# A gated scan, an up-projection by seven products and a down-projection: four kinds of GpSimd instruction at other places in its queue

## The reference, cut to what matters

```python
# x, f_logit: (2, 6080, 256)   lower_bound: (256,)   w_in: (256, 2048)   w_out: (2048, 256)
f = lower_bound + (1 - lower_bound) * sigmoid(f_logit)
h = f[:, t] * h + (1 - f[:, t]) * x[:, t]      # for t in range(6080); y[:, t] = h
u = y.reshape(12160, 256) @ w_in
g = where(u > 0, u, exp(min(u, 0)) - 1)        # ELU
out = g @ w_out                                # (12160, 256), float32
```

## Time and profile before

| | |
|---|---|
| median of 3 runs | 1010.96 us (1010.54 to 1011.62) |
| the profiled execution | 1011.16 us |
| its span in the profile | 1009.3 us |
| TensorE busy | 1003.2 us, 99% |
| ScalarE busy | 794.6 us, 79% |
| VectorE busy | 728.9 us, 72% |
| GpSimd busy | 632.9 us, 63% |
| TensorE's granted clock | full in all 40 slices |
| TensorE's share of the chain that ended last | 97% |
| GpSimd's low part of an operand made from `x` (L334), 33 of them | 1.16 / 1.30 / 1.76 us (least, median, most) |
| VectorE's `open_gate` (L584), longest | 1.56 us |
| GpSimd's idle time in block 0, ahead of ELU 30's low part | 5.60 us |
| distance of the same matmul in two blocks that follow each other | 83.34 us |

### The profile page before, as it was taken

One profiled execution on the slowest core, in us unless ns is written; L12 is line 12 of the kernel. 1 busy time (PEld: TensorE's weight loads), 2 busy tenths in 40 slices (PEclk: granted clock), 3 DMA queues, 4 the chain that ended last, 5 costly groups with the idle time before them and its releaser, 6 DMA issues.

```text
span 1009.3 us, 15356 instructions
## 1 busy us (share of the span) xinstructions
PE 1003.2 (99%) x4362; PEld 816.4 (81%) x4362; DVE 728.9 (72%) x913; ACT 794.6 (79%) x1427; POOL 632.9 (63%) x474
## 2 busy tenths in 40 slices
PE   8999999999999999999999999999999999999998
PEld 5788778888888888888888888888888888888997
DVE  6785886785787687688669669758867966875544
ACT  7997778877877777877787787787788778778775
POOL 2584897567557557656655755756675575566454
PEclk9999999999999999999999999999999999999999
DMA  7211102101201110210120120021021011000101
GB/s 271 63 32 43 54 1 74 53 1 52 73 0 32 41 51 0 73 52 0 55 70 0 42 60 24 6 66 52 0 62 62 0 42 60 12 0 5 40 1 37
DMA packets 23211, 41.88 MB, mean 41 GB/s; under 512 B 2704, under 2 KB 4240, under 8 KB 23184
## 3 DMA queue, kind: packets, MB, share of 16 engines
q1 hardware_dynamic: 22752, 41.04, 12.7%
q10 hardware_dynamic: 432, 0.53, 0.2%
HBM read 29.10 MB, written 12.45 MB: 41 GB/s over the span
## 4 chain that ended last, share of the span: by engine, by line
PE 97%; DVE 1%; issue 1%; DMA 1%; ACT 0%; ACTq 0%; DVEq 0%
PE acc L858 17%; PE acc L856 17%; PE acc L857 17%; PE h L828 14%; PE h L830 14%; PE h L832 13%; PE h L951 1%; PE h L952 1%; PE h L953 1%; DMA x<-value 1%; DVE x L599 0%; DVE x L591 0%; PE acc L952 0%; PE acc L953 0%; PE acc L951 0%
## 5 line engine op out<-in xcount | busy, mean ns | idle before, releaser
L314 POOL TENSOR_TENSOR g_lo<-e,g_hi 128x512 fp32r<-128x512 f32 (+1 forms) x384 | 517.3, 1356 | 370.7 <-ACT g_hi L452 370.4
L438 ACT ACTIVATE e<-h 128x512 f32<-128x512 f32 (+1 forms) x380 | 226.4, 596 | 163.6 <-PE h L832 128.3
L690 DVE SCALAR_TENSOR_TENSOR e<-e,h 128x512 f32<-128x512 f32 (+1 forms) x380 | 257.3, 677 | 80.0 <-ACT e L444 79.8
L858 PE MATMUL acc<-g_hi,w_out_lo 128*128 128x512 f32 (+1 forms) x768 | 301.9, 393 | 0.0
L856 PE MATMUL acc<-g_hi,w_out_hi 128*128 128x512 f32 (+1 forms) x768 | 301.0, 392 | 0.0
L857 PE MATMUL acc<-g_lo,w_out_hi 128*128 128x512 f32 (+1 forms) x768 | 299.7, 390 | 0.0
L452 ACT CAST g_hi<-e 128x512 fp32r<-128x512 f32 (+1 forms) x384 | 233.1, 607 | 22.3 <-DVE e L690 22.3
L444 ACT ACTIVATE e<-e 128x512 f32<-128x512 f32 (+1 forms) x384 | 242.1, 630 | 8.4
L828 PE MATMUL h<-a_hi,w_in_hi 128*128 128x512 f32 (+1 forms) x616 | 241.2, 392 | 0.3 <-DVE h L676 0.3
L830 PE MATMUL h<-a_lo,w_in_hi 128*128 128x512 f32 (+1 forms) x616 | 240.6, 391 | 0.0
L832 PE MATMUL h<-a_hi,w_in_lo 128*128 128x512 f32 (+1 forms) x616 | 238.8, 388 | 0.0
(11 more groups left out here) (64 smaller groups left out, 571.4 us busy)
## 6 DMA issues: line engine op xcount, KB each, us to landing
out<-out_sb SPq DMA_DIRECT2D x44, 256.0 KB, 2.1
gate<-forget_logit SPq DMA_DIRECT2D x43, 256.0 KB, 2.7
x<-value SPq DMA_DIRECT2D x43, 256.0 KB, 2.8
w_in_raw<-w_in SPq DMA_DIRECT2D x8, 256.0 KB, 6.4
w_out_raw<-w_out SPq DMA_DIRECT2D x8, 256.0 KB, 7.7
x<-value SPq DMA_DIRECT2D x4, 224.0 KB, 2.6
gate<-forget_logit SPq DMA_DIRECT2D x4, 224.0 KB, 2.5
out<-out_sb SPq DMA_DIRECT2D x4, 224.0 KB, 2.0
```

The lines of the kernel that those rows point to most:

```text
L314: nc.gpsimd.tensor_tensor(g_lo[:, t % RING, 0:w], e[:, t % TILES, 0:w], g_hi[:, t % RING, 0:w].bitcast(F32), ALU.subtract).then_inc(g_lo_r ...
L438: nc.scalar.activation(e[:, i, 0:w], bank_of(j, t)[:, 0:w], ACT.Relu, scale=-1.0).then_inc(r_ready, 1)
L690: nc.vector.scalar_tensor_tensor(e[:, t % TILES, 0:w], e[:, t % TILES, 0:w], -1.0, bank_of(j, t)[:, 0:w], ALU.add, ALU.max).then_inc(g_rea ...
L858: done = nc.tensor.matmul(bank, lo, g_hi[:, t % RING, 0:w], start=False, stop=closes)
```

## The change

Low part of the fourth operand: in every block from 1 on, GpSimd made it after the ELU low part of (q, i) = (0, C11) of the same block. Now it makes it after that of (7, C22) of the block before (t = 30), ahead of that of (7, C21).

Low parts of w_in for groups 2 to 7: the P1 to P3 pieces of groups 2 and 3 move from block 1 to block 0 (after t = 25 and 27), and the others take other places in block 1.

```diff
             def spare(j, par, q, i, last):
 
-                if (q, i) == (0, C11):
-                    rest(j, par, P4)
                 if last:
                     return
...
                     rest(j + 1, 1 - par, P6)
+                if (q, i) == (7, C22):
+                    rest(j + 1, 1 - par, P4)
 
             def second_spare(q, i):
 
                 at = (q, i)
-                if at in ((0, C12), (1, C11), (1, C22), (2, C12), (3, C12), (4, C12)):
-                    w_in_rest({(0, C12): 2, (1, C11): 3, (1, C22): 4, (2, C12): 5, (3, C12): 6, (4, C12): 7}[at],
-                              P1, P5)
-                if at in ((0, C22), (1, C12), (2, C11), (2, C22), (3, C22), (5, C12)):
-                    w_in_rest({(0, C22): 2, (1, C12): 3, (2, C11): 4, (2, C22): 5, (3, C22): 6, (5, C12): 7}[at],
+                if at in ((0, C22), (1, C12), (3, C22), (4, C21)):
+                    w_in_rest({(0, C22): 4, (1, C12): 5, (3, C22): 6, (4, C21): 7}[at], P1, P5)
+                if at in ((0, C11), (0, C12), (1, C11), (1, C22), (4, C12), (5, C12)):
+                    w_in_rest({(0, C11): 2, (0, C12): 3, (1, C11): 4, (1, C22): 5, (4, C12): 6, (5, C12): 7}[at],
                               P5, PRODUCTS)
...
                 rest_g(0, t)
                 if t in (18, 21):
                     rest(1, 1, {18: P1, 21: P2}[t])
+                if t in (25, 27):
+                    w_in_rest({25: 2, 27: 3}[t], P1, P5)
+                if t == 30:
+                    rest(1, 1, P4)
```

## The result

The changed kernel took 1009.52 us (median of 22 runs) where the kernel before took 1011.40 us beside it; the ratio is 0.9982, 95% interval 0.9975 to 0.9988. A second set of 11 runs gave 0.9983 (0.9974 to 0.9992). So the change wins 1.8 us of 1011, under 0.2%. Forecast were 1009.3 us and a gain of 1.64; "VectorE wins the race in group 2", the first rival, gave 1.91 and 1009.05. Both start from 1010.96 us, the median of three runs; the 22 runs beside the changed kernel have 1011.40. So the gains are to be compared and not the times. The interval, 1.2 to 2.5 us, holds 1.64 and 1.91 both: which of the two it was, only the trace tells.

What follows compares the result with a forecast made beforehand. TensorE, busy 99% of the span, bounds the kernel; only its waits can be won. 1.05 (fourth operand) + 0.59 (group 3 of block 1) = 1.64 us less, 1009.3 us against 1010.96; range 1008.5 to 1010.3.

Steps and rivals of the forecast that it cites:

- VectorE wins the race in group 2: Rival, block 1: VectorE's `weigh` begins ahead of GpSimd's ELU 7, so all 1.91 us go; 1009.05 us, chance 0.30.
- The ten waits are GpSimd's low part of the fourth operand: Ahead of P4 in group 0, blocks 1 to 10: TensorE's unnamed waits are for this GpSimd subtraction; moving it gives -1.05 us.
- It fits the idle time of 1.60 us and moves nothing: Steady blocks: the moved subtraction takes 1.30, at most 1.48, inside GpSimd's idle time before ELU 31; nothing behind it moves.
- Two pieces into block 0 cost nothing: Block 0: each piece takes 1.02 us in GpSimd's idle time and may hold a VectorE subtraction by up to 0.9; 0.
- The later pieces, 0: Block 1: pieces at (3, C22), (4, C12), (4, C21), (5, C12) meet over a microsecond of GpSimd idle time; cost 0.
- block 1's lateness only moves: Rival: pieces at (3, C22) or (4, C21) meet VectorE's backlog, or L676 stays late; only 1.05 won, 1009.9 us, chance 0.12.
- Group 3 of block 1, 0.59 us: P3's wait on `add_u4`: without a GpSimd piece between (1, C22) and (3, C22), `weigh` takes 0.68 us; -0.59 us.
- Group 2 of block 1, 0: P4's 0.27 us wait on `add_c22`: GpSimd's ELU 7 begins ahead of VectorE's `weigh`, as in block 3; nothing won.
- The hold lasts the whole instruction: Rival: `open_gate` comes 0.12 us later in group 2, loss there 0.39; gain 1.52, 1009.45 us, chance 0.05.
- the prediction's 0.89 us: Block 1, group 2: held `open_gate` truly ran from 0.89 us after GpSimd's begin, so from 116.56 after the change.

Runs made afterwards that it cites:

- the piece in group 2: Changed kernel with group 6's 128x384 low-part piece after (2, C12) and not after (3, C22); 1009.32 us in one run.
- The square of four: Changed kernel; with group 5's two pieces exchanged (1009.86 us); with group 6's 128x384 piece after (2, C12) (1009.32 us); with both edits (1010.55 us).
- the weights alone: Changed kernel with the fourth operand's low part back after (0, C11) of its own block; 1010.74 us, ratio 0.9995 to the kernel before.
- the operand one ELU later: Weights-only kernel with the fourth operand's low part after (0, C12) in place of (0, C11); 1067.1 us, ratio 1.055 to the kernel before.
- the operand last: Changed kernel with the fourth operand's low part after (7, C21), in block 0 after t = 31; 1009.55 us, ratio 0.9974 to the kernel before.

## Why the prediction was right, and where not

- *The ten waits are GpSimd's low part of the fourth operand.* Right. Moved alone it takes them away; made later, they grow to 4.0 us. Forecast 1.05 us; blocks are 0.106 us shorter, the ratio of that half is 0.9990.
- *It fits the idle time of 1.60 us and moves nothing.* Right: 1.30, with 0.34 left, `open_gate` unchanged. Even one place later it costs TensorE nothing. In block 0 the place was misread: the 5.60 us of idle time lie ahead of ELU 30's low part and the subtraction behind it, where 1.59 us are free and 0.33 were left.
- *Two pieces into block 0 cost nothing.* Right in the sum, with nothing to spare. Their price was mis-sized, 1.47 for 1.02 each, because VectorE held them; one VectorE subtraction was held by 0.82 (bound 0.9), all of the idle time named.
- *The later pieces, 0*, and the rival that block 1's lateness only moves. Right: no wait of TensorE after 30 us.
- *Group 3 of block 1, 0.59 us.* Right in size and sign, wrong in its cause. I put it on the piece in group 2, without which `weigh` was to take 0.68; it took 0.92. The square of four shows that this piece alone costs TensorE nothing. The loss needs the lateness of group 2 too, so curing either is enough; the change cured both. That the size came right with the cause half seen is luck.
- *Group 2 of block 1, 0.* This is the step that failed. I worked out the race as a tie, 118.36 against 118.37, and gave it to GpSimd by the precedent of block 3. It was a tie: the records begin at the same hundredth (118.60 in the first trace of the changed kernel), and VectorE passed. So it was in all six traces with the shorter piece ahead of ELU 6, at the times of each: both of the changed kernel and those of the weights alone, the operand one ELU later, the piece in group 2 and the operand last. Where GpSimd was ahead by 0.05 us or 0.28 it won, and block 3's 0.05 said nothing on a lead of 0. The 0.27 us came on top: 1.64 + 0.27 = 1.91 for the forecast 1.64, which is the first rival.
- *The hold lasts the whole instruction* (rival). Not seen, but the prediction's 0.89 us is wrong too. It reckons with 0.68 us for an `open_gate` that nothing holds, which is the duration of a free `weigh`. In the kernel before, GpSimd and then VectorE:

```profile
199.30 1.30 POOL L314 TENSOR_TENSOR g_lo<-e,g_hi 128x512 fp32r<-128x512 f32 x1 [1.08 <-ACT g_hi L452]
...
200.40 0.53 DVE L584 TENSOR_SCALAR gate<-gate,slope,offset 128x512 f32<-128x512 f32 x1
```

  An `open_gate` held by one such GpSimd instruction ends 1.57 to 1.59 us after GpSimd's begin wherever it was issued. This one ends at 200.93, 1.63 after it, so it wasn't held, and takes 0.53 free. Then the held ones really start 1.58 - 0.53 = 1.05 after GpSimd's begin. A held `weigh` (0.68 free) ends 1.85 after it, so it starts 1.17 after it. The forecast isn't touched, as it takes off 0.68 and adds it again. The rival's price is touched: by the whole instruction (1.29) `open_gate` in group 2 would have ended at 115.67 + 1.29 + 0.53 = 117.49 against 117.52 before, so the loss there would have stayed and not grown to 0.39. The rule of the Trainium skill, SBUF — State Buffer (Who interferes with whom), that the first to begin keeps the shared pair agrees with who won in each kernel here where one began first; its "whole instruction" is longer than the 1.05 and 1.17 us worked out here, of a record of 1.29.

By the spans, set against where block 0's first late product starts (29.18 before, 29.50 after), the gain is 1009.3 - 1007.8 + 0.3 = 1.8 us; the distances say 1.9. The 0.1 stays open.

## What to carry to other kernels

A wait that a profile marks only as issue, of the same length at the same place in every turn of a loop, is worth a look at what another engine ends 0.1 us ahead of it; moving that instruction later, and not only earlier, names the cause. Where an engine carries its lateness from stage to stage, losses don't add: the two edits of the square cost nothing in group 3 each and 0.6 us there together, so a loss read at the stage that pays says little on which stage to mend. When two engines come to a shared resource within a few hundredths, carry both outcomes with near equal chance, or choose sizes so that one is clearly first. And before taking a hold's length from a held instruction, look for the same instruction where nothing holds it, not for another one.

## What the runs showed of the hardware that was not expected

- A pause of 4.0 us on TensorE costs more than itself: some 1.0 us after the matmuls resume they go to half speed (granted clock 0.50, that is 1.2 GHz, in the table of block 1; distances of 0.43 us in all ten full blocks), for 3.4 to 3.7 us, and back to full after. That didn't happen after the pause of 3.0 us in the short last block, nor after any of the pauses under a microsecond.
- Of a weight load's lateness about 0.12 us isn't lost: 0.23 late lost 0.11, 0.40 lost 0.27, 0.70 lost 0.59, 4.04 lost 3.9.
- `open_gate` (one tile of SBUF, two scalars) is let in 1.05 us after GpSimd's begin, `weigh` (two tiles of SBUF) 1.17 us after it, both behind a GpSimd subtraction of 128x512 with a record of 1.29 us.
- Where both records begin at the same hundredth VectorE passed, six times of six (`weigh`, block 1). Where GpSimd's began 0.01 us ahead (130.25 against 130.26, block 1 of the kernel before) `open_gate` was held and took 1.56 us. The two cases differ in VectorE's instruction too, so what decides at so small a lead stays open.
